# Linear attention and two expert layers on one core: the causal mask's load issued one step later on ScalarE's queue, and TensorE's second scores ahead of its first state

## What is computed

```
state = gamma * state + k_t v_t^T          # B=2, H=8, D=64, S=768
y_t   = scale * q_t . state
x     = y as [B*S, H*D]                    # 1536 x 512
gate  = softmax(x @ w_gate); e = argmax    # 8 experts, capacity 384
x     = gate[e] * (relu(x @ w1[e]) @ w2[e])
h     = x @ w_in                           # 512 x 2048
out   = (P(h) / Q(h)) @ w_out              # P a cubic, Q with |h| and h^2
```

## Time and profile before

| | before |
|---|---|
| median of 3 runs | 537.37 us (536.67 to 538.62) |
| the profiled execution | 536.48 us |
| its span, first to last instruction | 534.6 us |
| PE busy | 525.8 us (98%) |
| PE weight loads busy | 439.0 us (82%) |
| VectorE busy | 425.0 us (79%) |
| ScalarE busy | 329.2 us (62%) |
| GpSimd busy | 76.6 us (14%) |
| moved by DMA | 72.26 MB, mean 135 GB/s |

### The profile page before, as it was taken

How to read it: one execution, slowest core, us unless ns; L and a number is a source line. 1 busy time by engine, 2 the same in 40 slices (tenths; PEclk the granted TensorE clock), 3 DMA queues, 4 the chain that set the end, 5 groups by cost and what they waited for, 6 DMA issues and landing times.

```text
span 534.6 us, 8737 instructions
## 1 busy us (share of the span) xinstructions
PE 525.8 (98%) x3209; PEld 439.0 (82%) x3209; DVE 425.0 (79%) x759; ACT 329.2 (62%) x508; POOL 76.6 (14%) x74
## 2 busy tenths in 40 slices
PE   7999999999999999999999999999999999999997
PEld 5887888888888888888788888888888888888885
DVE  3678788695856759577989999998888888787886
ACT  2454546484655747557869867657566566655652
POOL 2433342360101101003010010004000000200000
PEclk9999999999999999999999999999999999999999
DMA  9999959959958494903060000003000000200002
GB/s 192 229 269 234 281 200 394 398 145 390 380 232 307 146 332 149 397 25 99 23 217 1 1 21 20 1 1 115 4 21 20 1 0 2 78 1 0 0 1 79
DMA packets 65055, 72.26 MB, mean 135 GB/s; under 512 B 41202, under 2 KB 41714, under 8 KB 65012
## 3 DMA queue, kind: packets, MB, share of 16 engines
q1 hardware_dynamic: 58596, 57.96, 34.7%
q0 software_dynamic: 3136, 9.46, 5.2%
q10 hardware_dynamic: 3280, 4.28, 2.3%
HBM read 59.09 MB, written 12.60 MB: 134 GB/s over the span
## 4 chain that ended last, share of the span: by engine, by line
PE 94%; DMA 2%; DVE 1%; issue 1%; SPq 1%; POOL 1%; ACT 0%; POOLq 0%
PE up_low L953 7%; PE up_low L954 7%; PE up_low L955 7%; PE bank L955 6%; PE bank L953 6%; PE bank L954 6%; PE up_high L959 5%; PE up_low L959 5%; PE yrows L953 4%; PE yrows L954 4%; PE up_high L955 4%; PE up_high L953 4%; PE up_high L954 4%; PE yrows L955 4%; PE up_low L960 2%; PE up_high L960 2%
## 5 line engine op out<-in xcount | busy, mean ns | idle before, releaser
L880 DVE TENSOR_TENSOR T<-raw,T 128x1024 fp32r<-128x1024 f32 x60 | 71.5, 1221 | 34.0 <-ACT T L874 34.0
L874 ACT ACTIVATE T<-raw 128x1024 fp32r<-128x1024 f32 x60 | 60.5, 1070 | 32.4 <-PE bank L955 32.0
L953 PE MATMUL up_low<-x2H,T 128*128 128x512 f32 x176 | 69.3, 394 | 0.0
L955 PE MATMUL up_low<-x2H,T 128*128 128x512 f32 x176 | 68.6, 390 | 0.0
L954 PE MATMUL up_low<-x2L,T 128*128 128x512 f32 x176 | 68.6, 390 | 0.0
L1533 ACT ACTIVATE sq<-up_low 128x512 f32<-128x512 f32 x44 | 26.2, 595 | 64.5 <-PE up_low L955 64.3
L1554 DVE SCALAR_TENSOR_TENSOR wa<-sq,coef,wa 128x512 f32<-128x512 f32 x48 | 36.0, 749 | 28.7 <-ACT wa L1535 28.7
L953 PE MATMUL bank<-T,hL 128*128 128x512 f32 x128 | 50.6, 395 | 0.0
L955 PE MATMUL bank<-T,hH 128*128 128x512 f32 x128 | 49.9, 390 | 0.0
L954 PE MATMUL bank<-T,hH 128*128 128x512 f32 x128 | 49.9, 390 | 0.0
L1547 ACT ACTIVATE rc<-wa,cst 128x512 f32<-128x512 f32 x48 | 34.8, 725 | 20.5 <-DVE wa L1554 15.7
(11 more groups left out here) (205 smaller groups left out, 1231.2 us busy)
## 6 DMA issues: line engine op xcount, KB each, us to landing
raw<-in_moe_w_dram SPq DMA_DIRECT2D x14, 2048.0 KB, 11.0
raw<-in_moe_w_dram SPq DMA_DIRECT2D x8, 512.0 KB, 5.1
w_out_raw<-in_moe_w_out_dram SPq DMA_DIRECT2D x4, 1024.0 KB, 17.0
ybuf<-ysb ACTq DMA_DIRECT2D x15, 256.0 KB, 5.6
qin<-in_q_dram SPq DMA_DIRECT2D x12, 256.0 KB, 5.0
kin<-in_k_dram SPq DMA_DIRECT2D x12, 256.0 KB, 5.8
vin<-in_v_dram SPq DMA_DIRECT2D x12, 256.0 KB, 5.5
xbuf<-xt SPq DMA_DIRECT2D x12, 256.0 KB, 4.1
```

The lines of the kernel that those rows point to most:

```text
L874: e.activation(W[w][:, 0, cols], raws[par][:, w, cols], ACT.Copy).then_inc(r.wH[w], 1)
L880: e.tensor_tensor(W[w][:, 1, cols], raws[par][:, w, cols], W[w][:, 0, cols].bitcast(F32), ALU.subtract).then_inc(r.wL[w], 1)
L953: nc.tensor.matmul(out_, aL, bH, start=start, stop=False)
L955: return nc.tensor.matmul(out_, aH, bH, start=False, stop=stop)
```

## The change

Two edits in two queues. On PE, `pe_scores(1)` is called ahead of `pe_state(0)`. On ScalarE's queue, the load of the causal mask is no longer the third of the loads at the start; it is issued behind `act_evac_k(0)` and ahead of `act_evac_q(0)`. Semaphores, waits and all other instructions stay as they are.

```diff
@@ pe_first_tile
             pe_transpose_qk(0)
             pe_scores(0)
             pe_transpose_qk(1)
+            pe_scores(1)
             pe_state(0)
-            pe_scores(1)
             pe_values(0)
             pe_state(1)
@@ block.scalar
-            for a, b, s in ((lay["ident"][0], lay["ident"][1], s_ident), (lay["qdecay"][0], lay["kdecay"][1], s_ident),
-                            (lay["causal"][0], lay["causal"][1], s_causal)):
-                e.dma_start(cst[:, a:b], consts[:, a:b]).then_inc(s, 16)
+            for a, b in (lay["ident"], (lay["qdecay"][0], lay["kdecay"][1])):
+                e.dma_start(cst[:, a:b], consts[:, a:b]).then_inc(s_ident, 16)
             e.preload_act_table_set("natural_log_exp_and_others")
             act_evac_k(0)
+            a, b = lay["causal"]
+            e.dma_start(cst[:, a:b], consts[:, a:b]).then_inc(s_causal, 16)
             act_evac_q(0)
```

## The result

The changed kernel takes 540.66 us (median of 7 runs, 539.96 to 541.10) against 537.34 us for the kernel before beside it (7 runs, 536.65 to 538.62). The ratio is 1.0062, 95% interval 1.0051 to 1.0073: slower by 0.6%, 3.3 us. The forecast was 538.7 us, 1.35 us slower, so the sign was right and the size was less than half of what was measured. The result lies inside the forecast's range (537.0 to 541.5), between the times of its rivals (a), 539.8, and (b), 541.9. The profiled execution has a span of 539.2 us, 4.6 more than that of before.

A forecast was written before the change was run, and what follows sets the result against it. PE was taken as the bound, busy 525.8 of 534.6 us. Late mask and pe_state(0) 1.70, less 0.15 for keys and 0.20 for waits, gave +1.35 us on 537.37: 538.7 us, range 537.0 to 541.5.

The forecast's parts named there:

- (a): At VectorE's table subtraction: the causal table lands after about 10.9, POOL holds it until 12.08; +2.4 us, 539.8; chance 0.28.
- (b): In PE's gap before pe_scores(1): the clock falls, 3.2 us of PE work at half speed, 541.9 us; chance 0.10.
- What bounds the kernel: Whole kernel: PE is busy 525.8 of 534.6 us, so what the start loses or wins moves the end equally, barring 1.5 us of waits.
- The exposed wait: On PE: pe_scores(1) waits for the late mask until 12.70 with pe_state(0) behind it; tile 2's keys 1.70 us later.
- Issue and landing: On ScalarE's queue: causal load issued at 6.71 us, landing 4.1 us later at 10.8 (9.9 to 11.5).
- The meeting with POOL: At VectorE's subtraction, 10.85 us: landing inside POOL's first vs (to 10.94) costs nothing; inside the second, it is held until 12.08.
- Rival (c): At the start: landing in 3.2 us, the loss absorbed by earlier keys and a broken stall; 536.3 to 537.0 us; chance 0.15.
- the forecast's own case: Start of PE's queue: mask ends at 12.66, pe_scores(1) starts at 12.70, no clock fall; 538.7 us; chance 0.47.
- What comes back: After the late start: 0.15 us from earlier keys and 0.2 from later waits (bounds 1.5 back, 0.8 lost).
- the stall at 44.6: VectorE's comparison beside a POOL operation, PE waiting 0.8 us: may vanish with the change of phase; 0.2 us taken back.

The follow-up runs named there:

- the kernel with the mask first: Changed kernel with VectorE's three small tables behind the mask of tile 0 instead of ahead of it: 538.00 us, ratio 1.0028 against the kernel before.
- The fillers: Changed kernel with 10 matmuls of zeros between pe_transpose_qk(1) and pe_scores(1): 537.48 us, ratio 1.0028 against the kernel before.
- both cures: Changed kernel with VectorE's three tables behind the mask of tile 0 and 8 matmuls of zeros in PE's gap: 536.95 us, ratio 1.0015 against the kernel before.

## Why the prediction was right or wrong

**What bounds the kernel.** Right. By the table by stage PE is busy for all of 100 to 530 us in both kernels: behind 100 us nothing is made up, and what the first 19 us lose arrives at the end, less the 0.8 us.

**The exposed wait.** Right in mechanism: pe_scores(1) started 0.16 us behind the end of the mask, and pe_state(0) stood behind it. By the experiments the swap without the later load costs nothing, the later load without the swap 0.5%; with both, pe_state(0)'s 0.61 us no longer fill part of the gap.

**Issue and landing.** Right: issue 6.66 (6.71 was said), landing 4.1 us later (4.1), the subtraction at 10.73 (10.85). ScalarE's copy of the queries came at 7.18, not delayed by the issue.

**The meeting with POOL.** Wrong, and this is the first term that was mis-sized. The forecast had the landing inside the first vs operation, which would have cost nothing, and rival (a) inside the second. It took back 0.15 us for the keys because 64 KB left the front, but left POOL's vs where it was. The freed bytes brought v 0.49 us earlier (POOL's vs from 9.90 to 9.41) while the landing stayed at 10.7. This is more than scatter: in the eight profiles without the early mask load POOL's vs starts at 9.35 to 9.56, in the three with it at 9.78 to 9.90. The gap between the two operations moved from 10.94 to some 10.5, and the subtraction fell into the second one. That is rival (a), at a landing that the forecast had: the mask ended at 13.13 (12.66 forecast, 13.74 for (a)), and pe_scores(1) came at 13.29. In the sum, 12.70 - 11.61 = 1.09 becomes 13.29 - 11.61 = 1.68; with the 0.61 of pe_state(0) it is 2.29 instead of 1.70. The hold is 0.75 us of it, by the kernel with the mask first; without it pe_scores(1) would have come near 12.5. Rival (c) had a slip of the same kind on record: it put the subtraction at 9.95 "before POOL has the port", while POOL's vs began at 9.90 in the earlier trace rows.

**The clock.** Wrong in its chance. Rival (b) was given 0.10, and the fall came in 12 of 12 executions. It was priced at 3.2 us; in the first profile PE needed 18.90 - 13.29 = 5.61 us for the stretch that takes 3.20 at full speed, 2.4 us more, after a long fall, and in the second 17.83 - 13.20 = 4.63, 1.4 us more, after a short one. The two levels of the mask-first kernel give the price of a short fall in the time: 1.2 us.

The mistake was to take one gap of 0.91 us without a fall as evidence for a gap of 2.6 us or more. The runs show: a PE wait of 0.9 us in the kernel before, no fall on record in 56 of 57; waits of 2.1 and 2.2 us, 9 falls in 14 runs; 3.3 and 2.6, always. So the forecast's own case, a gap from 10.1 to 12.7, would most likely have had a fall too. It was a mistake as well to treat (a) and (b) as cases apart, since (a) makes the gap longer; at the forecast's prices the two together are 539.8 + 3.2 = 543.0, outside its range. What happened is (a) and (b) together, and that the time still lies inside is in part luck: the falls cost 1.4 or 2.4 us instead of 3.2, the mask came 0.6 us earlier than in (a), and more came back than was taken. Being slower by over 0.5% had been given 0.24.

The rule that the forecast set beside (b), from the Trainium skill, "TensorE: Matmul & The Clock Gate", "HAM oscillation", that waits for data between bursts of work bring the lower clock, pointed the right way where the one wait in the trace did not; the trace agrees with it in the direction only, for the page's example has longer waits than most of the gaps here. The fillers show that it is PE's idleness and not the lateness that costs this part: 1.0062 to 1.0028 with the mask as late as ever. Why the clock falls in some executions of one kernel and not in others stays open.

**What comes back.** 0.35 us was taken, 0.15 of it for the keys (they came 0.09 us earlier, 6.08 to 5.99; but 5.97 in the swap alone, with all loads in their place, so this is no more than scatter) and 0.2 for the stall at 44.6. The table of tiles gives 0.8 for the second, within the bounds of 1.5 and -0.8; that it comes back for a late start from whatever stands in the way, and not from this one stall, was not foreseen.

**The sum as measured.** Late mask 1.68 + 0.61 = 2.3; clock 1.4 to 2.4; given back 0.8: 2.9 to 3.9 us. Measured, 3.3 us on one chip and 2.9 on another. Without the clock, 1.5 us: the filled kernel measured 1.3. The span of the first profile is 4.6 us longer because it has the long fall, and a wait of 0.9 us for the copy of logits that is not in the first profile of before but is in its second.

## What to carry to other kernels

A wait that is covered by the order of another engine's program (here s_mk by pe_state(0)) is not free to be moved: before an instruction is put first in line, look at what all its waits would cost with the other edits in place. When a transfer is moved out of a crowd, work out anew everything that it makes earlier, since two things that used to miss each other can meet. And price an added gap on PE with its clock: what makes a gap longer also makes a fall of the clock more likely, so the two are priced together, and a few matmuls of zeros in the gap are a cheap test of it.

## What was not expected of the hardware

- The granted clock's column doesn't show the low level at the start. In the second profile of before, the table by stage shows 1.00 from 6 to 14 us while the same groups of matmuls take 1.09 and 2.08 us instead of 0.64 and 1.16. The 2.08 us are those of the same group in the changed kernel at a recorded 0.50. The second profile of the changed kernel has it too: 1.09 us for its first transposes, with 1.00 in the column. Durations of one shape tell the level where the record doesn't, and so a mean of 1.00 does not rule out a slow start; the two profiles of this one kernel differ by 2.55 us at tile 2, and the slower first groups are most of it.
- The clock can fall while PE works: at about 8.2 us in the profile with both cures, inside pe_scores(0), 0.2 us after it had started behind a wait of 0.69 us, and in two of the three profiled falls behind the long gap, 0.2 and 1 us after PE had started again.
- Of the falls, 3.4 us at the lower level (mask first, 12.4 to 15.8) cost PE 1.4 us over its normal stretch and 1.2 us of the kernel's time, and 6.8 us of it (changed kernel) cost 2.4.
- One wait stays open: in the first profile of after, and in the second of before, VectorE's copy L503 started some 1.2 us after all that it is seen to wait for had ended, near 73 to 76 us, and PE waited 0.9 to 1.0 us for it. No run here tells what held it.
